# Moving tensors within SBUF in a fused dynamic convolution and SwiGLU kernel: one unused tensor less, three tensors declared later

## The reference

```
# dynamic convolution: softmax over 7 taps per token and head, causal window of 7 tokens
w = exp(weight_gen - max(weight_gen, -1)); w = w / (sum(w, -1) + 1e-09)      # 4 x 4096 x 8 x 7
out = einsum('bshk,bskhg->bshg', w, x_unf)                                   # 8 heads of 24 columns
# gated MLP on the 16384 tokens
xn = x / sqrt(mean(x * x) + 1e-06) * rms_g
g = xn @ w_gate; silu = g / (1 + exp(-g)); val = xn @ w_val                  # 192 -> 1536, twice
result = (silu * val) @ w_out                                                # 1536 -> 192
```

## Time and profile before

| | |
|---|---|
| median of three runs | 1282.14 us (1281.68 to 1282.82) |
| the profiled execution | 1281.68 us, of which its span is 1279.7 us |
| busy in the span: PE, PEld | 1261.2 us (99%), 1180.4 us (92%) |
| busy in the span: DVE, ACT, POOL | 1002.0 us (78%), 662.6 us (52%), 44.7 us (3%) |
| DMA | 76.29 MB, mean 60 GB/s; 9 tenths busy in the first of 40 slices, 1 or 2 after |
| mean granted TensorE clock | 0.999 of full speed |

### The profile page before, as it was taken

The page is one execution under the profiler, slowest core; times in us unless marked ns, Lnnn a source line. Parts: engine busy times, 40 slices in busy tenths (PEclk is TensorE's granted clock), DMA queues, the critical chain, the costliest instruction groups (busy, mean ns, idle before and its releaser), DMA issues.

```text
span 1279.7 us, 32479 instructions
## 1 busy us (share of the span) xinstructions
PE 1261.2 (99%) x13544; PEld 1180.4 (92%) x13544; DVE 1002.0 (78%) x1516; ACT 662.6 (52%) x1426; POOL 44.7 (3%) x75
## 2 busy tenths in 40 slices
PE   8999999999999999999999999999999999999998
PEld 7988999999999899999989999999999999999997
DVE  7998888878787887888877777877877877877643
ACT  4554555565446555445564455554455554455543
POOL 1000000000000000000000000000000000000000
PEclk9999999999999999999999999999999999999999
DMA  9011321211211212212212112111122122121010
GB/s 292 40 43 27 97 67 44 69 58 56 62 47 56 69 45 69 57 38 69 69 45 68 47 50 69 53 61 57 44 64 69 45 69 57 39 69 39 14 38 14
DMA packets 19734, 76.29 MB, mean 60 GB/s; under 512 B 3212, under 2 KB 4876, under 8 KB 19464
## 3 DMA queue, kind: packets, MB, share of 16 engines
q1 hardware_dynamic: 18764, 72.78, 18.8%
q10 hardware_dynamic: 828, 1.47, 0.5%
HBM read 38.06 MB, written 12.58 MB: 40 GB/s over the span
## 4 chain that ended last, share of the span: by engine, by line
PE 90%; DVE 4%; issue 2%; ACT 2%; DMA 1%; ACTq 0%; POOL 0%; DVEq 0%
PE up_ps L796 57%; PE out_ps L836 22%; PE out_ps L840 10%; DVE h L683 1%; DMA raw<-in_moe_w_val 1%; DVE prod L224 1%; DVE y L226 1%; DVE h_lo L703 1%; PE up_ps L745 1%; ACT silu L469 1%; ACT L469 0%; ACT L449 0%; PE up_ps L750 0%; DMA taps<-in_weight_gen 0%; DVE last L635 0%
## 5 line engine op out<-in xcount | busy, mean ns | idle before, releaser
L796 PE MATMUL up_ps<-xT,w_hi 64*128 64x512 f32 x4608 | 779.7, 390 | 4.3 <-DVE h L683 3.5
L796 PEld LDWEIGHTS up_ps<-xT,w_hi 64*128 64x128 f32 x4608 | 481.2, 184 | 51.4 <-issue 6.7
L796 PE MATMUL up_ps<-xT,w_lo 64*128 64x512 f32 x2304 | 476.1, 387 | 0.0
L836 PE MATMUL out_ps<-wo,h_hi 64*128 64x384 f32 x3072 | 456.0, 354 | 5.5 <-DVE last L635 1.6
L484 ACT ACTIVATE h_hi<-h 128x512 fp32r<-128x512 f32 x384 | 242.4, 631 | 338.8 <-DVE h L683 332.2
L683 DVE TENSOR_TENSOR h<-up_ps,silu 128x512 f32<-128x512 f32 x384 | 264.4, 688 | 194.0 <-ACT silu L469 191.7
L840 PE MATMUL out_ps<-wo,h_lo 64*128 64x192 f32 x3072 | 413.3, 247 | 0.0
L469 ACT ACTIVATE silu<-up_ps 128x512 f32<-128x512 f32 x384 | 228.5, 595 | 238.9 <-PE up_ps L796 232.2
L836 PEld LDWEIGHTS out_ps<-wo,h_hi 64*128 64x128 f32 x3072 | 322.6, 184 | 11.2 <-DVE last L635 2.4
L840 PEld LDWEIGHTS out_ps<-wo,h_lo 64*128 64x128 f32 x3072 | 327.3, 187 | 3.7
L703 DVE TENSOR_TENSOR h_lo<-h,h_hi 128x512 fp32r<-128x512 f32 x384 | 263.1, 685 | 34.9 <-ACT h_hi L484 34.6
(11 more groups left out here) (75 smaller groups left out, 301.5 us busy)
## 6 DMA issues: line engine op xcount, KB each, us to landing
x_buf<-in_x SPq DMA_DIRECT2D x30, 960.0 KB, 4.7
xT<-xT SPq DMA_DIRECT2D x90, 256.0 KB, 3.8
result<-last SPq DMA_DIRECT2D x32, 384.0 KB, 2.3
taps<-in_weight_gen SPq DMA_DIRECT2D x1, 3136.0 KB, 20.7
raw<-in_moe_w_gate SPq DMA_DIRECT2D x3, 384.0 KB, 8.6
raw<-in_moe_w_val ACTq DMA_DIRECT2D x3, 384.0 KB, 10.4
last<-in_moe_w_out SPq DMA_DIRECT2D x1, 1152.0 KB, 18.0
x_first<-in_x SPq DMA_DIRECT2D x2, 384.0 KB, 7.4
```

The lines of the kernel that those rows point to most:

```text
L796: mm = nc.tensor.matmul(ps[:, banks, :], w[rows, s, cols], xT[rows, t, s, part, :], start=(at == 0), stop=ends)
L836: nc.tensor.matmul(out_ps[:, j, 0:2 * D], h_hi[rows, g % HB, cols], wo[rows, g, :, :].rearrange("p a d -> p (a d)"), start=(g == 0 and k < ...
```

## The change

The tensor `spare` (216 numbers, 864 bytes in each partition) is no longer declared; nothing read or wrote it. The declarations of xT, h_hi and h_lo move down, xT behind xn, h_hi and h_lo behind h. Nothing else is different.

```diff
         gains = sb("gains", [P, SLOTS])
-        spare = sb("spare", [P, 216])
         w_hi = sb("w_hi", [P, SLOTS, F], F32R)
         w_lo = sb("w_lo", [P, SLOTS, F], F32R)
         wo = sb("wo", [P, FB, 2, D], F32R)
-        xT = sb("xT", [P, 2, SLOTS, 2, N], F32R)
-        h_hi = sb("h_hi", [P, HB, N], F32R)
-        h_lo = sb("h_lo", [P, HB, N], F32R)
         ident = sb("ident", [P, P])
...
         xn_a, xn_b = (v.rearrange("p (j d) -> p j d", j=J) for v in (xn[:, 0:J * DA], xn[:, J * DA:]))
+        xT = sb("xT", [P, 2, SLOTS, 2, N], F32R)
 
         silu = sb("silu", [P, 2, N])
         h = sb("h", [P, 2, N])
+        h_hi = sb("h_hi", [P, HB, N], F32R)
+        h_lo = sb("h_lo", [P, HB, N], F32R)
```

## The result

The changed kernel takes 1302.67 us (median of 4 runs, 1302.23 to 1303.92) against 1282.29 us before (4 runs): ratio 1.0158, 95% interval 1.0146 to 1.0172. That is 20.4 us slower than before. The forecast was 1282.2 us with a range of 1277 to 1292, so the result lies outside it, and the chance given to slower was 24%.

The account below looks back on a forecast made before the run. The prediction took TensorE's stream of matmul pairs to bound the kernel. Its sum was 1281.68 + 0 + 0 + 0; from the median of 1282.14, rounded up for the start, it forecast 1282.2 us, range 1277 to 1292.

Parts of the forecast that it names:

- What bounds the kernel: Whole kernel: one stream of TensorE matmul pairs, 227 ns a hidden pair; hidden pairs and projection steps make 1220 us.
- Same instructions, waits, bytes: All engines and queues: only byte positions in SBUF differ, so instruction count, bytes moved and queues give exactly 0.
- Term (a): TensorE's matmul operands losing their 1 KB alignment: taken as 0, upper bound 7.7 us.
- rival 1: Slower, L796, L836, L840: operands that straddle a block cost time, from 2.6 us up to 7.7 us (1289.9); chance 17%.
- Term (b): xT, h_hi and h_lo moving beside tensors ScalarE and VectorE work on: taken as 0, bound 4.6 us.
- Term (c): DMAs starting at other addresses, copies of xT and first load of the taps: 0, bound 0.3 us for the taps.
- Rival 2: Slower: writes beside h_hi, h_lo and xT hold up TensorE's loads and streams; 1286.8, or 1297 with hidden pairs; chance 7%.
- Rival 3: Faster: aligned loads and streams collide in step, moving them apart helps; 1278.7 at 1 ns a pair, 1236 at most; 13%.
- the 14 ns between the halves: Hidden pairs: second half starts some 14 ns after the first, said to account for 227 ns against 213.3.
- the slower rivals: Rival 1 and rival 2, the two cases of a slower kernel; chance together 24%.

Follow-up runs that it names:

- experiment 1: Kernel before the change with only the unused 864-byte tensor removed, declarations in their old order: 1283.21 us, ratio 0.9993.
- experiment 2: Changed kernel with the 864 bytes back and 736 more ahead of xT, so TensorE's operands begin on multiples of 1024: 1282.91 us, ratio 0.9999 to before.
- 7: Changed kernel with one unused tensor of 224 bytes ahead of xT: 1282.77 us, ratio 1.0001 to before.
- distance 256: Kernel before the change with xT alone moved 256 bytes on from where the weights stand: 227 ns a hidden pair; its total time is not in the text.

## Why the prediction was wrong

- *What bounds the kernel.* Right, and it is why the loss is whole: the stream of pairs has no slack, and 645 ns more a tile are 20.6 us more at the end.
- *Same instructions, waits, bytes.* Right: the waits fell by 1.4 us, the other engines' busy times did not move beyond 1.4 us.
- *Term (a), the step that failed.* "An unaligned moving operand costs nothing visible ... I take 0." The term measured 20.4 us, 2.6 times its upper bound of 7.7. The question put was whether an operand stands on a boundary, and to that 0 is the answer (experiment 1). It was the wrong question: what counts is the distance between two operands that TensorE reads together, and in L796, L836 and L840 that was 0 in before and 288 (32 modulo 256) in the changed kernel. Of the 20.6 us that the tiles add up to, 17.0 are in the hidden matmuls (532 ns a tile) and 3.6 in the projections (113 ns). The rows used do hold other distances: in the earlier trace rows ident is loaded against ident streamed (distance 0) at 0.85 ns a column and against y and xn (128 and 288) at 0.84. But that is half the column rate, and of matmuls of 128 against 384 columns. No cost shows there, while at 0.44 ns a column the distance costs 3%. The prediction named this gap under rival 1 and still set its bound without a full-rate row: the 7.7 us are a spread of 6 in 951 ns among VectorE's products, carried over to TensorE's 1220 us, and say nothing of TensorE.
- *Term (b).* Right, 0: experiment 2. The Trainium skill's "SBUF — State Buffer", "Who interferes with whom", was cited for it. The runs agree for the other engines, whose tensors beside xT, h_hi and h_lo cost nothing in experiment 2; they do not for TensorE against itself, where that section has a port for the streamed operand and one for the loads, independent of each other: 6 ns a pair hang on how the two stand.
- *Term (c).* Right as far as can be seen: copies land in 3.8 us, taps in 3.14 for 3.11. The first hidden matmul came at 24.66 for 24.05 us, but in kernels as fast as before (experiments 1, 2, 7 and distance 256) it came at 25.7 to 27.8, so the start varies by more than that.
- *Rival 1* had the side and the sign of what would be seen (longer distances, waits unchanged), but the wrong cause, and a price too low. *Rival 2* is out. *Rival 3* had the right pair of operands, "in step, since all start alike", and the wrong sign: in step is the good case. Its counter-argument, the 14 ns between the halves, was wrong as well (experiment 1).
- The range ended at 1292 because both prices of the slower rivals were taken from spreads of a few ns (6 among VectorE's products, 3 among TensorE's loads) in rows that did not contain the effect.

What stays open: why a distance of 0 modulo 256 is good, why 64 is less bad and 240 worse than the rest, and why one displaced load in three costs about as much as three. That the load and the stream meet somewhere inside SBUF or on TensorE's way to it fits, but was only argued; that the other engines have no part was tested by moving them along (1, 2) and not by taking them away.

## What to carry to other kernels

Where TensorE is the bound and runs matmuls as here (pairs of 64 rows, four-byte numbers, 0.44 ns a column, a load for each), lay out the tensor that is loaded and the tensor that is streamed so that they begin at the same place modulo 256 bytes. A pad of 224 bytes is worth 1.6% here, and alignment as such nothing. Other shapes and types were not tried. A change that only moves tensors is not free: look at the distance between tensors read together, not at each tensor's own address. And a price at full rate is not bounded by rows at half rate or of another engine: the bound was 7.7 us and 20.4 were measured.

## What was not expected of the hardware

- The distance of two SBUF operands modulo 256 bytes changes the start-to-start distance of the pairs of 64x512 matmuls from 227 to 233 ns (235 at worst), with the same instructions, the same clock and no longer waits.
- The halves of a pair (gate and value) can start from 3 to 150 ns apart, by tile or by run (medians of 3 and 37 ns in tiles 12 and 20 of the changed kernel, up to 150 in experiment 1), without any effect on the rate: 233.4 ns a pair in both those tiles.
- The first hidden matmul started between 24.05 and 27.8 us in single executions of kernels whose medians are within 1 us, so the start is no place to look for small gains with one trace.
